# Loading a feed-forward layer's first weights a piece per attention pair, and the rest in one block behind the first batch's last v

## The chip, the cores and the metric

The program runs on one core of a Trainium2 chip. The metric is device time in microseconds; the time before is the median of 3 runs. Beside the runs there is one profiled execution, and every row below is from it. The engines are named as the profile names them: PE (matrix products and transposes; PEld is its weight load), DVE (vector), ACT (scalar), POOL, and SP, which issues all DMAs here; an engine's name with q behind it is its sequencer.

## The reference

Three layers follow one another on 4 x 576 tokens of width 512, all in float32:

```python
# attention: 4 batches x 8 heads, 576 tokens, head width 64
out_d     = softmax(q_d @ k_d.T / 8) @ v_d        # q, k, v averaged over 4 tokens each
out_local = softmax(mask(q @ k.T / 8)) @ v        # |i - j| < 4
x = repeat(out_d, 4) + out_local                  # -> [2304, 512]
# gated feed-forward, width 1536
x = (sigmoid(x @ w_gate) * (x @ w_val)) @ w_out
# soft mixture: 8 experts x 4 slots
logits = x @ phi;  d = softmax over tokens;  c = softmax over slots
slots = d.T @ x;  slots_out = relu(slots @ w1[e]) @ w2[e];  out = c @ slots_out
```

## The kernel before

**Staging.** The kernel's program is one list of steps, `head` and then `body`; every engine walks the same list and does its own part of each step, in that order. Attention works on pairs of heads (16 pairs, 4 to a batch). The head handles the four pairs of the first batch, in turns, and begins on pair 4; the body runs the gated layer over 18 tiles of 128 tokens, three chunks of 512 columns each (steps `gate (i, c)` and `val (i, c)`, 12 matrix products each), with the attention of the other batches, step by step, between them. Behind the body comes the mixture of experts.

**Steps of a pair p.** `Q0`, `Q1`, `K0`, `K1` transpose q and k; `S0`, `S1` are the local scores and `Sd` the pooled ones; `mx`, `ex`, `norm` (and `mxd`, `exd`, `norm_d`) the softmax; `PT` and `PdT` transpose probabilities; `pool_V` adds up v on POOL; `PVd`, `PV0` to `PV2` are the products with v. `PV` of pair p also waits until that pair's local v has landed in `vloc`.

**Weights of the gated layer.** w_gate and w_val are loaded in 12 pieces of 512 KB (`load_pieces` into `w_raw`, 128 partitions x 2 x 512 float32). Pieces 0 to 3 are chunk 0 (two for gate, two for val), 4 to 7 chunk 1, 8 to 11 chunk 2. Each is split into a high part (`w_hi`, a copy on ACT) and a low part (`w_lo`, a subtraction on DVE). `gate (0, c)` waits for the first 4c + 2 low parts, `val (0, c)` for 4c + 4.

**w_out.** It is loaded in 12 pieces of 256 KB into four stages (`load_wo_piece`, L498); `WT f` transposes piece f on PE (L909) and copies it on ACT, `GP f` multiplies it with phi, `GS` gathers four of them. Piece f + 4 may be loaded when `WT f` is done.

**SP's queue.** SP walks the step list as well (`sync_step`): after `Q1` and `K1` of a pair it loads q and k of the next, after `pool_V` the v to be pooled (`v4`), after `PV2` the local v of the next pair (six DMAs, L468 to L474). A load stands in SP's order behind all that is issued, or waited for, ahead of it. The extra loads of the head are in the function at the end of the kernel:

```python
if s == ("S1", 0):
    load_pieces(sp, range(0, 3))
if s[0] == "PV2" and s[1] < 3:
    load_pieces(sp, range(3 * s[1] + 3, 3 * s[1] + 6))
```

So pieces 0 to 2 come ahead of q and k of pair 2, pieces 3 to 5 behind the local v of pair 1, 6 to 8 behind that of pair 2, 9 to 11 behind that of pair 3. Pieces 0 to 5 of w_out are loaded within the first pair's steps.

The step lists of the turns (TURN, FIRST_TURNS, HEAD_TURN, LAST_TURN) give the order in the head; `program_steps` writes the body. In the head a turn splits one piece (`w_hi` and `w_lo`); the last turn has two more `w_hi`. The body opens with xs 0 (tile 0 split into high and low parts), WT 2, WT 3, w_lo 4, w_lo 5, w_hi 6, w_hi 7, mx0 and mx1 of pair 4, gate (0, 0).

Of the kernel before, what the change touches and what calls it, by code (L numbers as in the profile page):

```python
# [30 lines left out]
               PV0 PV1 PV2""")  # L31
HEAD_TURN = """S0+ S1+ w_hi norm norm_d PT0 PT1 PT2 mx0+ mx1+ PdT0 PdT1 Sd+ PVd pool_V+ Q++ ex+ K++ mxd+ exd+ w_lo
               PV0 PV1 PV2"""
LAST_TURN = """S0+ S1+ w_hi norm norm_d PT0 PT1 PT2 PdT0 PdT1 w_lo PVd w_hi w_hi PV0 PV1 PV2"""

UNITS = ("Q0", "Q1", "K0", "K1", "S0", "S1", "Sd", "PdT0", "PdT1", "PVd", "PT0", "PT1", "PT2", "PV0", "PV1", "PV2",
         "WT", "GP", "GS", "TR", "LG", "LS", "ELT", "SL")
# [19 lines left out]
def program_steps(tiles, chunks, groups, batch_tokens, pairs, heads_of, w_pieces, wo_pieces):  # L57

    turns = [*zip((-2, -1, 0), FIRST_TURNS)] + [(p, HEAD_TURN) for p in range(1, heads_of - 1)] + \
            [(heads_of - 1, LAST_TURN)]
    head = attention_steps(turns, 0, heads_of + 1)
    done = set(head)
    att = [s for s in attention_steps([(p, TURN) for p in range(heads_of - 2, pairs)], heads_of, pairs) if s not in done]
    f0 = sum(s[0] == "GP" for s in head)
    split = {name: sum(s[0] == name for s in head) for name in ("w_hi", "w_lo")}
    start = [("xs", 0), ("WT", f0), ("WT", f0 + 1)]
    for n in range(split["w_lo"], 8):
        if n >= split["w_hi"]:  # L70
            start.append(("w_hi", n))
        if n < 6:
            start.append(("w_lo", n))
    start += [("mx0", heads_of), ("mx1", heads_of)]
    att = [s for s in att if s not in start]


    t0 = tiles - 3
    ff = [(name, (i, c)) for i in range(t0) for c in range(chunks) for name in ("gate", "val")]
    ff += [(name, (i, 0)) for i in range(t0, tiles) for name in ("gate", "val")]  # L80
    for c in range(1, chunks):
        ff += [("gate", (t0, c)), ("val", (t0, c)), ("gate", (t0 + 1, c)), ("gate", (t0 + 2, c)), ("val", (t0 + 1, c)),
               ("val", (t0 + 2, c))]
    place_of = {s: n for n, s in enumerate(ff)}


    after = {n: [] for n in range(len(ff) + 12)}

    def put(n, *steps):
        after[n] += steps  # L90


    marks = [(0, 3)]
    for b in range(1, pairs // heads_of):
        first_tile = b * batch_tokens // P
        k = att.index(("PV2", heads_of * (b + 1) - 1)) + 1
        marks.append((k, place_of[("gate", (first_tile, 0))] - 3))
    marks.append((len(att), marks[-1][1]))
    for (k0, n0), (k1, n1) in zip(marks, marks[1:]):
        for k in range(k0, k1):  # L100
            put(n0 + (k - k0) * (n1 - n0) // max(k1 - k0, 1), att[k])

    for n in range(6, w_pieces):
        if n >= 8:
            put(n // 2 - 4, ("w_hi", n))
        put(n // 2 - 3, ("w_lo", n))

    for f in range(f0, wo_pieces):
        n = f - f0 + 1
        if f >= f0 + 2:  # L110
            put(n - 1, ("WT", f))
        put(n, ("GP", f))
        if f % 4 == 3:
            put(n + 1, ("GS", f // 4))
    for i in range(1, tiles):

        put(place_of[("gate", (i, 0))] - 2 if i < t0 else place_of[("gate", (t0 - 1, 0))] + i - t0, ("xs", i))
    for i in range(t0):
        for c in range(chunks):
            put(place_of[("val", (i, c))] + 1, ("TR", (i, c)))  # L120
    for g, (first, size) in enumerate(groups):
        n = place_of[("val", (first + size - 1, chunks - 1))]
        if first + size < t0:
            for at, name in ((2, "LG"), (3, "LS"), (5, "ELT"), (6, "SL")):
                put(n + at, (name, g))

    last_c, g = chunks - 1, len(groups) - 3
    n = place_of[("gate", (t0, 0))]
    for at, *those in ((1, ("LG", g)), (2, ("LS", g)), (3, ("ELT", g), ("TR", (t0, 0)), ("SL", g)), (5, ("TR", (t0 + 2, 0)))):
        put(n + at, *those)  # L130
    for c in range(1, last_c):
        n = place_of[("gate", (t0, c))]
        put(n + 2, ("TR", (t0, c)))
        put(n + 5, ("TR", (t0 + 2, c)))
    n = place_of[("gate", (t0, last_c))]
    for at, *those in ((2, ("TR", (t0, last_c))), (3, ("LG", g + 1)), (4, ("LS", g + 1), *[("TR", (t0 + 1, c)) for c in range(chunks)]),
                       (5, ("ELT", g + 1), ("LG0", g + 2), ("TR", (t0 + 2, last_c)), ("SL", g + 1)),
                       (6, ("LG", g + 2)), (7, ("LS", g + 2)), (8, ("ELT", g + 2)), (9, ("SL", g + 2))):
        put(n + at, *those)
    body = []  # L140
    for n, s in enumerate(ff):
        body.append(s)
        body += after[n]
    for n in range(len(ff), len(ff) + 12):
        body += after[n]
    return head, start + body
# [36 lines left out]
def build(nc, q, k, v, w_gate, w_val, w_out, phi, w1, w2, out):  # L183
# [26 lines left out]
    FK = FF // P  # L210
# [16 lines left out]
    head, body = program_steps(TILES, FC, GROUPS, S, PAIRS, HP, len(w_pieces), FK)  # L227
# [12 lines left out]
    with ctx:  # L240
# [3 lines left out]
        def sem(name):  # L244
            return ctx.enter_context(nc.semaphore(name))
# [71 lines left out]
        WO_STAGES = KT  # L317
# [52 lines left out]
        w_hi = sem("w_hi")  # L370
        w_lo = sem("w_lo")
# [57 lines left out]
        def wait_unit(eng, s):  # L429
            eng.wait_ge(unit_ready, at[s][0] + 1)  # L430
# [57 lines left out]
        def load_pieces(sp, of):  # L488
            for i in of:
                c, m, kk = w_pieces[i]  # L490
                src = (w_gate, w_val)[m][kk * P:(kk + WK) * P, c * CW:(c + 1) * CW].rearrange("(k p) n -> p k n", p=P)
                sp.dma_start(w_views(i)[0], src).then_inc(w_in[i], 16)


        def load_wo_piece(sp, f):
            if f >= WO_STAGES:
                wait_unit(sp, ("WT", f - WO_STAGES))
            sp.dma_start(wo_stage[f % WO_STAGES], w_out[f * P:(f + 1) * P, :]).then_inc(wo_in[f % WO_STAGES], 16)  # L498
# [47 lines left out]
        def sync_step(sp, s):  # L546
            name, arg = s
            if name == "Q1" and arg + 1 < PAIRS:
                wait_unit(sp, s)
                load_pair_qk(sp, arg + 1, "q")  # L550
            elif name == "K1" and arg + 1 < PAIRS:
                wait_unit(sp, s)
                load_pair_qk(sp, arg + 1, "k")
            elif name == "PV2" and arg + 1 < PAIRS:
                wait_unit(sp, s)
                load_v_local(sp, arg + 1)
            elif name == "WT" and arg + WO_STAGES < FK:
                load_wo_piece(sp, arg + WO_STAGES)
            elif name == "pool_V" and arg + 1 < PAIRS:
                sp.wait_ge(vd_done, arg + 1)  # L560
                load_v_pooled(sp, arg + 1)
# [567 lines left out]
        @block.sync  # L1129
        def _(sp):  # L1130
            load_pair_qk(sp, 0, "q")
            load_pair_qk(sp, 0, "k")
            for f in range(2):
                load_wo_piece(sp, f)
            sp.dma_start(phi_sb[:, :, :], phi.rearrange("(k p) s -> p k s", p=P)).then_inc(phi_in, 16)
            for s in head:
                sync_step(sp, s)
                if s == ("K1", 0):
                    load_v_pooled(sp, 0)
                    for f in range(2, WO_STAGES):  # L1140
                        load_wo_piece(sp, f)
                    load_v_local(sp, 0)

                if s == ("S1", 0):
                    load_pieces(sp, range(0, 3))
                if s[0] == "PV2" and s[1] < 3:
                    load_pieces(sp, range(3 * s[1] + 3, 3 * s[1] + 6))
            for s in body:
                sync_step(sp, s)

            wait_free(sp, *[(f"PV{u}", PAIRS - 1) for u in range(3)])
            load_wo_tail(sp)
            for i in range(FIRST):
                wait_place(sp, place_of_tile(i))
                load_tile(sp, i)
            for i in range(FIRST, N_TILES):
                n = place_of_tile(i)
                if n < WO_SLOTS:
                    sp.wait_ge(sin_ready, 1)
                else:  # L1160
                    gone = n - WO_SLOTS
                    sp.wait_ge((w1_used, w2_used)[gone // 2 % 2], gone // 4 + 1)
                load_tile(sp, i)
            for i in range(TILES):
                sp.wait_ge((out_evac_a, out_evac_v)[i % 2], i // 2 + 1)
                sp.dma_start(out[i * P:(i + 1) * P, :], outs[:, i, :]).then_inc(out_saved, 16)
            sp.wait_ge(out_saved, 16 * TILES)
# [76 lines left out]
```

## Time and profile before

| what | us |
|---|---|
| median of 3 runs | 601.73 (600.63 to 601.77) |
| the profiled execution, its own time | 600.79 |
| its span | 599.0 |
| PE busy in the span | 550.9 (92%) |
| DVE busy | 224.4 (37%) |
| ACT busy | 200.1 (33%) |
| POOL busy | 100.7 (17%) |
| chain that ended last: PE | 83% of the span |
| chain that ended last: DMA | 6% |

The span is what the profile's own clock covers; 1.8 us of the execution's time lie around it. A line of the timeline has the start, the duration, the engine, the line of the kernel, the operation, the tile written and read, the count of instructions merged, and in brackets the idle time of the engine before it and what ended that.

### The profile page before, as it was taken

Reading aid. Unit: us, or ns where it says so; the run is one execution under the profiler, and the core shown is the slowest. Engines: PE = TensorE matmul, PEld = TensorE weight load, DVE = VectorE, ACT = ScalarE, POOL = GpSimd, SP = SyncE. Lnnn points to the kernel's source line nnn. Section 1 sums busy time; section 2 is a strip of 40 time slices with the busy share of each in tenths; the row PEclk is TensorE's granted clock in tenths of the full one; section 3 lists DMA queues with packets and bytes.
Section 4 is the critical chain, followed back from the end, with each engine's and each line's share of the span. In section 5 each row is a group of like instructions: output and inputs, shape, how many; then the busy total and the mean of one; then the engine's idle time right before and its main releaser. Section 6 shows DMA issues by size and latency. Waiting matters only on the chain.

```text
span 599.0 us, 11279 instructions
## 1 busy us (share of the span) xinstructions
PE 550.9 (92%) x4486; PEld 413.8 (69%) x4486; DVE 224.4 (37%) x500; ACT 200.1 (33%) x514; POOL 100.7 (17%) x171
## 2 busy tenths in 40 slices
PE   5686899999999999999999999999999999968963
PEld 4575776776878778777777877787787777833422
DVE  3487752525535252434326243542212221130003
ACT  4355653343433424242333334133223211130103
POOL 7655012232221212112120302110000000000000
PEclk9779799999999999999999999999999999999988
DMA  9879522211311111202120110101703256589958
GB/s 201 209 198 230 177 80 69 65 40 42 82 40 42 41 42 36 46 20 53 27 48 20 50 33 21 23 3 34 267 1 109 103 207 257 202 313 394 399 197 315
DMA packets 86707, 70.97 MB, mean 118 GB/s; under 512 B 61312, under 2 KB 65920, under 8 KB 86656
## 3 DMA queue, kind: packets, MB, share of 16 engines
q1 hardware_dynamic: 86656, 70.25, 38.0%
q8 instruction: 36, 0.59, 0.4%
q14 instruction: 15, 0.12, 0.1%
HBM read 65.52 MB, written 4.72 MB: 117 GB/s over the span
## 4 chain that ended last, share of the span: by engine, by line
PE 83%; DMA 6%; DVE 5%; issue 2%; ACT 2%; SPq 1%; DVEq 0%
PE gateb L946 26%; PE valb L946 25%; PE unitb L954 4%; PE unitb L903 3%; DMA ew_low<-in_moe_w_dram 3%; PE unitb L859 3%; PE unitb L866 2%; PE unitb L968 2%; PE unitb L985 2%; PE unitb L894 2%; PE unitb L874 2%; DMA qtok<-in_q_dram 2%; PE unitb L1029 2%; PE unitb L881 1%; PE unitb L909 1%
## 5 line engine op out<-in xcount | busy, mean ns | idle before, releaser
L946 PE MATMUL gateb<-w_hl,xhl 128*128 128x512 f32 x648 | 162.8, 400 | 0.0
L946 PE MATMUL valb<-w_hl,xhl 128*128 128x512 f32 x648 | 162.1, 399 | 0.0
L946 PEld LDWEIGHTS gateb<-w_hl,xhl 128*128 128x128 f32 x648 | 118.7, 189 | 33.0 <-issue 9.1
L946 PEld LDWEIGHTS valb<-w_hl,xhl 128*128 128x128 f32 x648 | 118.6, 188 | 23.9 <-issue 0.2
L665 ACT ACTIVATE hid<-gateb 128x512 f32<-128x512 f32 x54 | 32.3, 598 | 170.9 <-PE gateb L946 170.9
L785 DVE SCALAR_TENSOR_TENSOR hid<-hid,valb 128x512 f32<-128x512 f32 x54 | 37.1, 688 | 128.7 <-PE valb L946 128.6
L583 POOL TENSOR_TENSOR vd<-v 72x256 f32<-72x256 f32 x16 | 12.7, 793 | 172.9 <-PE unitb L887 168.0
L594 ACT ACTIVATE hT<-unitb 128x512 f32<-128x512 f32 x54 | 32.0, 597 | 21.2 <-PE unitb L954 21.2
L768 DVE TENSOR_TENSOR xraw<-unitb,outd 128x192 f32<-128x192 f32 x43 | 15.0, 356 | 55.8 <-PE unitb L903 55.6
L954 PE MATMUL unitb<-ident,hid 128*128 128x128 f32 x216 | 33.3, 278 | 2.5 <-DVE hid L785 1.7
L954 PEld LDWEIGHTS unitb<-ident,hid 128*128 128x128 f32 x216 | 24.3, 140 | 7.7 <-issue 4.1
L903 PE MATMUL unitb<-probT,vloc 70*64 70x64 f32 x516 | 22.2, 231 | 4.6 <-DMA vloc<-in_v_dram 4.6
L903 PEld LDWEIGHTS unitb<-probT,vloc 70*64 70x64 f32 x516 | 18.2, 141 | 11.7 <-issue 10.9
L894 PE MATMUL unitb<-ident,prob 128*70 128x128 f32 x123 | 20.5, 282 | 3.9 <-DVE prob L747 3.9
L777 DVE TENSOR_TENSOR xhl<-xraw,xhl 128x512 fp32r<-128x512 f32 x18 | 12.8, 710 | 28.6 <-ACT xhl L594 28.6
L866 PEld LDWEIGHTS unitb<-kT,qT 64*64 64x64 f32 x488 | 17.8, 143 | 5.3 <-issue 5.0
L866 PE MATMUL unitb<-kT,qT 64*64 64x70 f32 x488 | 20.5, 235 | 0.3 <-ACT kT L594 0.3
L752 DVE COPY probT<-unitb 70x384 f32<-70x384 f32 x13 | 7.2, 553 | 34.5 <-PE unitb L894 34.5
L578 POOL TENSOR_TENSOR kd<-kd,kT 128x144 f32<-128x144 f32 x32 | 19.2, 599 | 2.5
L594 ACT ACTIVATE qT<-unitb 128x384 f32<-128x384 f32 (+1 forms) x30 | 11.1, 414 | 24.7 <-PE unitb L859 24.7
L578 POOL TENSOR_TENSOR qd<-qd,qT 128x144 f32<-128x144 f32 x32 | 18.9, 590 | 2.5
L575 POOL TENSOR_TENSOR qd<-qT 128x144 f32<-128x144 f32 x16 | 9.3, 580 | 59.3 <-ACT qT L594 59.2
(174 smaller groups left out, 666.7 us busy)
## 6 DMA issues: line engine op xcount, KB each, us to landing
ew_low<-in_moe_w_dram SPq DMA_DIRECT2D x19, 1024.0 KB, 13.7
ew_high<-in_moe_w_dram SPq DMA_DIRECT2D x13, 1024.0 KB, 7.9
qtok<-in_q_dram SPq DMA_DIRECT2D x32, 144.0 KB, 2.8
ktok<-in_k_dram SPq DMA_DIRECT2D x32, 144.0 KB, 3.0
v<-in_v_dram SPq DMA_DIRECT2D x32, 144.0 KB
out_dram<-outs SPq DMA_DIRECT2D x18, 256.0 KB, 3.0
vloc<-in_v_dram SPq DMA_DIRECT2D x32, 112.0 KB
xraw<-in_moe_w_out_dram SPq DMA_DIRECT2D x12, 256.0 KB, 3.6
```

The costliest lines, as they stand in the source:

```text
L578: nc.gpsimd.tensor_tensor(dst, dst, src[j], ALU.add).then_inc(step if j == 2 else done, 1)
L594: return nc.scalar.activation(dst, src, ACT.Copy, scale=scale)
L665: nc.scalar.activation(hid[:, i % NH, c * CW:(c + 1) * CW], gateb[n % 2][:, :], ACT.Tanh, scale=0.5)\
L768: nc.vector.tensor_tensor(dst.rearrange("p (g j) -> p g j", j=POOL), ub[:, 0:3 * QT].rearrange("p (g j) -> p g j", j=POOL), up, ALU.add).t ...
L777: nc.vector.tensor_tensor(xhl[:, arg % NX, 1, :, :], xraw[:, :, tok:tok + P], xhl[:, arg % NX, 0, :, :].bitcast(F32), ALU.subtract).then_i ...
L785: nc.vector.scalar_tensor_tensor(out=here, in0=here, scalar=1.0, in1=valb[n % 2][:, :], op0=ALU.add, op1=ALU.mult).then_inc(hid_done, 1)
L859: last = nc.tensor.transpose(ub[:, (t - t0) * TT:(t - t0 + 1) * TT], tok[:, t, :, :].rearrange("p h d -> p (h d)"), ident[0:TT, 0:TT])
L866: last = mm(ub[rows, (t - t0) * KW:(t - t0 + 1) * KW], qT[rows, t * QT:(t + 1) * QT], kT[rows, key_start(t):key_start(t) + KW], start=True ...
L894: last = nc.tensor.transpose(ub[0:KW, j * P:(j + 1) * P], prob[:, arg % 2, 3 * u + j, :], ident[:])
L903: last = mm(ub[rows, j * QT:(j + 1) * QT], vloc[:, t, h, :], probT[:, t, h * QT:(h + 1) * QT], start=True, stop=True)
L946: last = mm(bank[:, :], xhl[:, i % NX, x, kk, :], w_hl[:, c, m, w, kk, :], start=j == 0, stop=j == len(order) - 1)
L954: last = nc.tensor.transpose(ub[:, j * P:(j + 1) * P], hid[:, i % NH, f * P:(f + 1) * P], ident[:])
```

## The change

The head loads fewer weights ahead of its attention, and the rest in one block:

- Behind S1 of pair 0 come pieces 0 and 1; behind PV2 of pairs 0 and 1 one piece each (2 and 3). Each is loaded a turn before the turn that splits it.
- Behind PV2 of pair 2, and so behind the local v of pair 3, come pieces 4 to 11 and pieces 2 to 5 of w_out, in the order 4, 5, wo 2, 6, 7, wo 3, 8, 9, wo 4, 10, 11, wo 5. Pieces 2 to 5 of w_out are no longer loaded within the first pair's steps.
- The last turn of the head has one w_hi, no longer three. The body opens with xs 0, w_hi 4, w_lo 4, w_hi 5, w_lo 5, mx0, mx1. Pieces 6 and 7 are split behind gate (0, 0), 8 and 9 behind val (0, 0), 10 and 11 behind gate (0, 1).
- WT 2 and WT 3 go behind gate (0, 0) and behind val (0, 0).

```diff
-LAST_TURN = """... PdT0 PdT1 w_lo PVd w_hi w_hi PV0 PV1 PV2"""
+LAST_TURN = """... PdT0 PdT1 w_lo PVd PV0 PV1 PV2"""
...
-    start = [("xs", 0), ("WT", f0), ("WT", f0 + 1)]
-    for n in range(split["w_lo"], 8):
-        if n >= split["w_hi"]:
-            start.append(("w_hi", n))
-        if n < 6:
-            start.append(("w_lo", n))
+    split = sum(s[0] == "w_lo" for s in head)
+    start = [("xs", 0)]
+    for n in range(split, 6):
+        start += [("w_hi", n), ("w_lo", n)]
...
     for n in range(6, w_pieces):
-        if n >= 8:
-            put(n // 2 - 4, ("w_hi", n))
-        put(n // 2 - 3, ("w_lo", n))
+        put(n // 2 - 3, ("w_hi", n), ("w_lo", n))
...
-        if f >= f0 + 2:
-            put(n - 1, ("WT", f))
+        put(n - 1, ("WT", f))
...
-            elif name == "WT" and arg + WO_STAGES < FK:
+            elif name == "WT" and 2 <= arg < FK - WO_STAGES:
                 load_wo_piece(sp, arg + WO_STAGES)
...
                 if s == ("K1", 0):
                     load_v_pooled(sp, 0)
-                    for f in range(2, WO_STAGES):
+                    load_v_local(sp, 0)
+
+                if s == ("S1", 0):
+                    load_pieces(sp, range(0, 2))
+                if s[0] == "PV2" and s[1] < 2:
+                    load_pieces(sp, range(s[1] + 2, s[1] + 3))
+                if s == ("PV2", 2):
+                    load_pieces(sp, range(4, 6))
+                    for f in range(2, 6):
                         load_wo_piece(sp, f)
-                    load_v_local(sp, 0)
-
-                if s == ("S1", 0):
-                    load_pieces(sp, range(0, 3))
-                if s[0] == "PV2" and s[1] < 3:
-                    load_pieces(sp, range(3 * s[1] + 3, 3 * s[1] + 6))
+                        if f < 5:
+                            load_pieces(sp, range(2 * f + 2, 2 * f + 4))
```

## Rows read from the trace of the kernel before

**Rows 1.** The page, part 2: busy tenths and granted clock in 40 slices.

```profile
PE   5686899999999999999999999999999999968963
...
PEclk9779799999999999999999999999999999999988
```

**Rows 2.** The chain that ended last, in order of time: start, us, what.

```profile
16.64 9.93 DMA qtok<-in_q_dram
...
48.39 2.80 DMA vloc<-in_v_dram
...
60.45 1.65 DMA vloc<-in_v_dram
...
553.61 16.73 DMA ew_low<-in_moe_w_dram
```

**Rows 3.** Timeline from 18 to 27 us: SP's k load, PE around its gap.

```profile
18.48 6.14 SPq L463 DMA_DIRECT2D ktok<-in_k_dram  x2
...
21.96 0.95 PE L874 MATMUL valb<-kd,qd 64*64 64x144 f32 x12 [0.41 <-POOL kd L578]
...
26.70 1.15 PE L859 MATMUL unitb<-ident,qtok 96*128 96x96 f32 x6 [3.79 <-DMA qtok<-in_q_dram]
```

**Rows 4.** Windows of 2 us: busy us of each engine (instructions), PE's clock, DMA share, GB/s.

```profile
18.00:20.00 2.00, 2.00 (x20) 1.51 (x16) 1.35 (x3) 0.39 (x1) 1.84 (x4) 0.51 1.07 394
...
22.00:24.00 2.00, 0.92 (x12) 0.65 (x12) 1.65 (x3) 0.82 (x1) 0.00 (x0) 1.00 1.18 149
...
28.00:30.00 2.00, 2.00 (x28) 1.78 (x28) 0.26 (x1) 2.00 (x9) 1.42 (x3) 0.50 0.37 120
...
52.00:54.00 2.00, 1.84 (x57) 1.63 (x52) 1.95 (x5) 1.18 (x3) 1.84 (x5) 1.00 1.05 406
...
62.00:64.00 2.00, 1.77 (x34) 1.80 (x35) 0.54 (x2) 0.38 (x1) 0.00 (x0) 0.50 0.77 264
```

**Rows 5.** Timeline from 44 to 62 us: SP's loads ahead of local v, and PE.

```profile
44.17 1.09 SPq L463 DMA_DIRECT2D ktok<-in_k_dram  x2
...
48.39 0.32 SPq L474 DMA_DIRECT2D vloc<-in_v_dram  x1
...
51.32 1.27 PE L903 MATMUL unitb<-probT,vloc 70*64 70x64 f32 x36 [1.21 <-DMA vloc<-in_v_dram]
...
54.05 3.02 SPq L463 DMA_DIRECT2D ktok<-in_k_dram  x2
...
58.12 0.71 PE L887 MATMUL unitb<-probdT,vd 72*64 72x144 f32 x8 [0.54 <-ACT probdT L594]
...
60.45 0.32 SPq L474 DMA_DIRECT2D vloc<-in_v_dram  x1
...
62.23 0.91 PE L903 MATMUL unitb<-probT,vloc 70*64 70x64 f32 x12 [3.40 <-DMA vloc<-in_v_dram]
```

**Rows 6.** Timeline from 64 to 84 us: PE at the body's start.

```profile
64.35 1.97 PE L909 MATMUL unitb<-ident,xraw 128*128 128x128 f32 x8
...
65.97 3.83 PE L946 MATMUL gateb<-w_hl,xhl 128*128 128x512 f32 x12
...
76.11 0.66 PE L909 MATMUL unitb<-ident,xraw 128*128 128x128 f32 x4
...
83.19 3.01 PE L946 MATMUL gateb<-w_hl,xhl 128*128 128x512 f32 x12
```

**Rows 7.** The tile w_raw: min/median/max ns, first and last start.

```profile
L594 ACT ACTIVATE w_hl<-w_raw x12: 1042/1051/1097, 21.8 to 73.2; 128x1024 fp32r<-128x1024 f32 x12
L773 DVE TENSOR_TENSOR w_hl<-w_raw,w_hl x12: 1206/1218/1765, 23.5 to 76.6; 128x1024 fp32r<-128x1024 f32 x12
```

**Rows 8.** Timeline: the same 36 score products in two turns.

```profile
30.90 2.37 PE L866 MATMUL unitb<-kT,qT 64*64 64x70 f32 x36
...
41.14 1.32 PE L866 MATMUL unitb<-kT,qT 64*64 64x70 f32 x36 [0.30 <-ACT kT L594]
```

**Rows 9.** A window of 15 us in the head, columns as in Rows 4.

```profile
30.00:45.00 15.00, 13.13 (x182) 11.18 (x179) 13.17 (x28) 8.03 (x23) 7.63 (x12) 0.73 0.73 198
```

More of the change, by code:

```diff
@@ L33 @@
                PV0 PV1 PV2"""
-LAST_TURN = """S0+ S1+ w_hi norm norm_d PT0 PT1 PT2 PdT0 PdT1 w_lo PVd w_hi w_hi PV0 PV1 PV2"""
+LAST_TURN = """S0+ S1+ w_hi norm norm_d PT0 PT1 PT2 PdT0 PdT1 w_lo PVd PV0 PV1 PV2"""
 UNITS = ("Q0", "Q1", "K0", "K1", "S0", "S1", "Sd", "PdT0", "PdT1", "PVd", "PT0", "PT1", "PT2", "PV0", "PV1", "PV2",
@@ L66, in program_steps @@
     f0 = sum(s[0] == "GP" for s in head)
-    split = {name: sum(s[0] == name for s in head) for name in ("w_hi", "w_lo")}
-    start = [("xs", 0), ("WT", f0), ("WT", f0 + 1)]
-    for n in range(split["w_lo"], 8):
-        if n >= split["w_hi"]:
-            start.append(("w_hi", n))
-        if n < 6:
-            start.append(("w_lo", n))
+    split = sum(s[0] == "w_lo" for s in head)
+    start = [("xs", 0)]
+    for n in range(split, 6):
+        start += [("w_hi", n), ("w_lo", n)]
     start += [("mx0", heads_of), ("mx1", heads_of)]
@@ L1139, in _ @@
                     load_v_pooled(sp, 0)
-                    for f in range(2, WO_STAGES):
-                        load_wo_piece(sp, f)
                     load_v_local(sp, 0)
                 if s == ("S1", 0):
-                    load_pieces(sp, range(0, 3))
-                if s[0] == "PV2" and s[1] < 3:
-                    load_pieces(sp, range(3 * s[1] + 3, 3 * s[1] + 6))
+                    load_pieces(sp, range(0, 2))
[4 more added lines that the diff above has]
+                    for f in range(2, 6):
+                        load_wo_piece(sp, f)
+                        if f < 5:
+                            load_pieces(sp, range(2 * f + 2, 2 * f + 4))
             for s in body:
```

## The prediction

> **What bounds the kernel now.** I began with the page's slices, to see where PE is not the bound. A slice is 15 us. From the sixth to the thirty-fifth PE is full at the full clock; it has holes in the first five (75 us), where the granted clock also drops, and in the last five [rows 1]. The change touches the first 85 us only. The later work follows PE: where PE reaches the body earlier, all behind it moves by as much, the loads of the experts' weights too, since SP issues them when PE's work has freed their places; the wait of 16.73 us for them at the end moves along and does not shrink [rows 2]. So the question is how much earlier PE gets through the head and the body's first chunk.
>
> Then I read the chain in order of time for what it says of DMA in the head. It names three transfers: q of pair 2, and the local v of pairs 2 and 3 [rows 2]. On PE's timeline they are three gaps: 3.79 us up to 26.70 [rows 3], 1.21 us up to 51.32 and 3.40 us up to 62.23 [rows 5]. The windows say what the DMA engines did ahead of each gap. At 18 to 20 us they moved 394 GB/s: weights, in rows of 2 KB. At 22 to 24 us they were as busy and moved 149, the 256-byte rows of q and k [rows 4]. So q of pair 2 stood behind weights that nobody needed yet, and SP's issue of k behind it took 6.14 us where 1.09 is enough for the same two DMAs in a later turn [rows 3, 5]. I read that as back-pressure of the full queue.
>
> **First gap.** Taken from in front of q of pair 2: pieces 2 to 5 of w_out (4 x 256 KB) and weight piece 2 (512 KB), 1.57 MB. At 394 GB/s [rows 4] that is 4.0 us. q landed at 16.64 + 9.93 = 26.6 [rows 2], so it would land at 22.6; PE is done with the work ahead at 21.96 + 0.95 = 22.9 [rows 3]. The gap goes nearly whole. Five issues leave SP's queue there too, which only helps. Bounds: 0 (if q is slow for another reason, as its 149 GB/s might say) and 3.79. I take 3.7: weights moved at 394 just ahead of it. What is late next is nothing on PE: the v to be pooled lands earlier as well, and the local v of pair 0 stands ahead of the pieces.
>
> **Second gap.** Pieces 3 to 5 had been moved well before the local v of pair 2 was issued, and 6 to 8 are issued behind it. It landed some 2.6 us after its last issue (48.39 + 0.32 to 51.32) [rows 5], and that issue stands behind pooled v, q and k on SP, which start only when POOL is done. The change takes none of that away. Bounds 0 and 1.21; I take 0.
>
> **Third gap.** Here pieces 6 to 8 (1.5 MB) go out just ahead of v, q and k: 406 GB/s at 52 to 54 us [rows 4], and the k issue takes 3.02 instead of 1.09 [rows 5]. With one piece there the 1.9 us go, so the last v issue ends at 58.8 instead of 60.77 and the data, 1.5 to 2.6 us behind it as in the two cases, is there at 60.3 to 61.4. PE is ready at 58.12 + 0.71 = 58.83. So 1.5 or more of the gap stays and about 1.9 goes. Bounds 0 and 3.40; I take 1.9.
>
> **WT 2 and WT 3.** Eight transposes leave the place ahead of the first gate product: the gate starts 65.97 - 64.35 = 1.62 us sooner. They come back between gate and val at the full clock, 0.66 for four as the profile models it [rows 6], or down to 0.45 as far as the next product lets them overlap: 0.9 to 1.3 us. Gain 0.3 to 0.7; I take 0.5.
>
> **The splitting.** DVE's part is eight w_lo of 1.22 us behind the head as before. ACT gets two more w_hi, 2.1 us, in the body [rows 7]. w_hi 4 and 5 lie under the first gate product (3.83 us [rows 6]), where ACT has only xs 0 to finish. Then ACT's order is: tanh of gate (0, 0), w_hi 6, w_hi 7, the copy of WT 2, w_hi 8 and 9, copies of GP 2 and WT 3, tanh of gate (0, 1). Queued behind the two w_hi is the copy that GP 2 on PE waits for: it ends about 0.7 + 2.1 + 0.6 = 3.4 us after gate (0, 0); PE comes to GP 2 after WT 2 and val (0, 0), 0.7 + 2.9 = 3.6 us. This is covered by 0.2 us only. Without cover it costs what is missing, up to 2.1. I take a loss of 0.4.
>
> **The block.** Eight pieces and four of w_out are 5.24 MB, 12.9 us at 406 GB/s [rows 4]. Its issue starts behind the local v of pair 3, at 58.8 less the 3.7 gained before, so at 55.1; some 2 us later it moves. Piece 5 is there at about 60, piece 7 (2.36 MB) at 63, piece 9 at 66, piece 11 at 70. PE starts gate (0, 0) at 65.97 - 3.7 - 1.9 - 1.6 = 58.8, so ACT, done with xs 0 at about that time, asks for piece 4 at 58.7, for 6 at 63.3, 7 at 64.4, 8 at 66, 11 at 72. Piece 4 lands near 58.5. All are just in time, and the small waits fall under gate (0, 0). The local v of pair 4 and all later loads now queue behind the block on SP; pair 4 needs its v only behind the whole of tile 0. Cost 0; bounds 0 and the slower rival below.
>
> The Trainium skill's page DMA: Bandwidth & Descriptors, section Where 436 GB/s comes from, says that transfers from HBM are bound at about 358 GB/s for a core; by that the block would take an estimated 14.6 us and piece 11 would come at 72, still in time, so the sum would not change by more than some tenths. The windows here differ, at 394 and 406 GB/s over 2 us, and the trace decides.
>
> **The clock.** Behind the first gap the granted clock is 0.50, the lower level of 1.2 GHz (28 to 30 us), and behind the third again (62 to 64 us) [rows 4]. The same 36 products took 2.37 us there and 1.32 at the full clock [rows 8], so one turn could win over 1 us on these alone. But in that turn DVE is busy 13.17 of 15 us [rows 9], so it would soon be the bound; and with a gap of 1.5 us left ahead of PV of pair 3 the clock may stay low there. Bounds: a loss of 1 (the drop falls on another stretch) to a gain of 3. I take 0.8, nearer to nothing because DVE is close.
>
> The Trainium skill's page TensorE: Matmul & The Clock Gate, Part 1, says that the throttled state is the default and only activity releases it. The rows agree as far as the low level stands behind each long gap. By that rule alone both stretches would come at full speed once the gaps are gone, which is the rival of a larger gain below.
>
> **Sum.** 3.7 + 0 + 1.9 + 0.5 - 0.4 + 0 + 0.8 = 6.5 us. From the profiled execution's own 600.79 that gives 594.3; it lay 0.94 below the median of the runs, so the forecast of the median is 595.2.
>
> **Rivals.**
> - *Only the first gap goes* (chance 0.14). SP's chain POOL, pooled v, q, k, local v sets when PV can start, and a PE that comes earlier just waits longer there; the body gives back a part. For it: the second gap stands without any piece in the way. Against it: the first gap moves the start of that chain too. 3.7 less 0.5 to 2.1: 598.5 to 600.1.
> - *Slower* (0.06). The block comes too late and ACT, in order, holds up PE. If it moved at the pace of the small rows, 149 to 200 GB/s [rows 4], piece 11 would land near 57 + 5.0 MB / 0.175 = 86; the copies and the softmax of pair 4 stand behind its split on ACT, and gate (0, 2), at 83.19 before [rows 6], would start near 90: 6 to 7 us slower, about 608. It decides below some 225 GB/s, where piece 11 lands near 79. Against it: pieces alone on the queue have moved at 394 to 406.
> - *The gain is spent again* (0.07). Both GP 2 and GP 3 wait for ACT and the low clock comes back in other turns: within 0.2% of 601.7, the resolution of a measurement of this kernel.
> - *Larger gain* (0.06). Full clock from 27 us on and at the first gate: 3 us instead of 0.8, the second gap gone too: 588 to 591.5.
>
> The forecast itself, 592 to 598, has 0.67. Faster by over 0.2% (below 600.5) is the forecast, the larger gain and the first rival: 0.87; no change 0.07, slower 0.06. The range from 589.8 to 600.1 takes in the first rival and half of the larger gain, and leaves out about 0.16.
>
> **What would show it.** After the change the gap ahead of the transposes of q of pair 2 is under 0.5 us, and no k issue in the head is over 2 us. The gap ahead of PV of pair 3 is 1 to 2 us, that of pair 2 about as before. gate (0, 0) starts near 59 and gate (0, 2) near 77, 6 to 7 us ahead of 83.19; from there to the end everything is shifted by the same amount. The 2 KB rows run in one stretch of 13 us at about 400 GB/s from 56 us on. Wrong it would be if ACT's w_hi in the body wait for their pieces, if PE waits at GP 2 or GP 3 for over 1 us, or if the low clock covers as much of the head as before.

## The result and the profile after

| | us |
|---|---|
| before, 4 runs | 601.31 (600.63 to 601.77) |
| changed kernel, 4 runs | 596.64 (594.65 to 597.21) |
| ratio, 95% interval | 0.9917 [0.9892, 0.9943] |
| profiled execution of before, of the changed kernel | 600.79, 594.65 |

The change makes the kernel 4.7 us faster by the medians, 6.1 us by the two profiled executions; that of the changed kernel was the fastest of its four runs. The forecast was 595.2 from a sum of 6.5 us.

The page of the changed kernel, part 2, PE and its clock by slices of 15 us:

```profile
PE   6787998999999999999999999999999999968963
...
PEclk9697999999999999999999999999999999999988
```

Against [rows 1] the slices 1, 2, 4 and 5 are a tenth fuller, the seventh is a tenth emptier, and from the eighth on PE's line is the same digit for digit. What the change does, it does in the first 77 us. The timeline there, with the lines that answer to [rows 3, 5, 6] (PE, and of SP the k loads, the pooled v of pair 4 and the last DMA for the local v of pair 3):

```profile
18.64 1.06 SPq L457 DMA_DIRECT2D ktok<-in_k_dram  x2
...
23.20 0.97 PE L868 MATMUL valb<-kd,qd 64*64 64x144 f32 x12 [1.75 <-POOL kd L572]
...
24.09 1.22 PE L853 MATMUL unitb<-ident,qtok 96*128 96x96 f32 x6
...
36.90 1.32 PE L860 MATMUL unitb<-kT,qT 64*64 64x70 f32 x36 [0.25 <-ACT kT L588]
...
46.77 1.27 PE L897 MATMUL unitb<-probT,vloc 70*64 70x64 f32 x36 [1.01 <-DMA vloc<-in_v_dram]
...
47.34 0.74 SPq L475 DMA_DIRECT2D v<-in_v_dram  x2
...
49.10 1.92 SPq L457 DMA_DIRECT2D ktok<-in_k_dram  x2
...
54.56 0.32 SPq L468 DMA_DIRECT2D vloc<-in_v_dram  x1
...
54.80 0.71 PE L881 MATMUL unitb<-probdT,vd 72*64 72x144 f32 x8 [0.54 <-issue]
...
56.35 0.57 PE L897 MATMUL unitb<-probT,vloc 70*64 70x64 f32 x12 [0.84 <-DMA vloc<-in_v_dram]
...
58.18 4.57 PE L940 MATMUL gateb<-w_hl,xhl 128*128 128x512 f32 x12 [0.55 <-ACT xhl L588]
...
66.22 0.66 PE L903 MATMUL unitb<-ident,xraw 128*128 128x128 f32 x4
...
77.00 3.01 PE L940 MATMUL gateb<-w_hl,xhl 128*128 128x512 f32 x12
```

PE no longer waits for q of pair 2, and the issue of k has gone from 6.14 us to 1.06. But PE now waits 1.75 us just ahead of that place, for POOL's pooled k (`kd`) of pair 1: a smaller gap has taken the place of the first. The gap at pair 2's v stands (1.01 us), that at pair 3's has shrunk from 3.40 to 0.84. The body then takes longer from gate (0, 0) to gate (0, 2). Put together by the starts of PE's work (scores of the next pair, then the two gates), with a second profile of the changed kernel from another execution (run c below):

| stretch up to | before | changed | changed, second profile |
|---|---|---|---|
| scores of pair 2 | 30.90 | 28.33 | 26.08 |
| scores of pair 3 | + 10.24 | + 8.57 | + 9.93 |
| scores of pair 4 | + 11.38 | + 11.07 | + 9.96 |
| gate (0, 0) | + 13.45 | + 10.21 | + 12.34 |
| gate (0, 2) | + 17.22 = 83.19 | + 18.82 = 77.00 | + 18.95 = 77.26 |

6.19 us are gained at gate (0, 2), and 6.1 at the end of the span. The two profiles of one kernel split them differently, by up to 2.3 us at a stretch, and agree at gate (0, 0) within 0.13 us; run c below takes that up.

The weights' block, in windows with the columns of [rows 4]:

```profile
62.00:64.00 2.00, 2.00 (x13) 1.64 (x12) 1.97 (x4) 1.22 (x2) 0.00 (x0) 1.00 1.02 390
64.00:66.00 2.00, 2.00 (x14) 1.40 (x15) 1.93 (x4) 1.76 (x3) 0.00 (x0) 1.00 1.05 400
66.00:68.00 2.00, 2.00 (x18) 1.59 (x15) 2.00 (x3) 1.43 (x2) 0.00 (x0) 1.00 1.05 386
```

It moves in one stretch near the rate that was assumed, beside a full PE: from 58 to 68 us 387 GB/s on average in this profile, 383 in the second.

### The profile page after: what moved, and what is told of

Same layout as the page of the kernel before. It is cut to its first block, busy times and chain, and to the rows that moved or that the text cites. A ratio compares the mean times of both kernels' runs of the same rounds, so it can differ in the third digit from the quotient of the medians.

```text
span 592.9 us, 11279 instructions
## 1 busy us (share of the span) xinstructions
PE 549.3 (93%) x4486; PEld 412.9 (70%) x4486; DVE 224.3 (38%) x500; ACT 200.1 (34%) x514; POOL 101.5 (17%) x171
## 4 chain that ended last, share of the span: by engine, by line
PE 83%; DMA 5%; DVE 4%; issue 2%; ACT 2%; POOL 1%; SPq 1%; POOLq 0%; ACTq 0%; DVEq 0%
PE gateb L940 26%; PE valb L940 25%; PE unitb L948 4%; PE unitb L897 3%; DMA ew_low<-in_moe_w_dram 3%; PE unitb L853 3%; PE unitb L860 2%; PE unitb L962 2%; PE unitb L979 2%; PE unitb L888 2%; PE unitb L868 2%; PE unitb L1023 2%; PE unitb L875 2%; PE unitb L881 1%; PE gateb L1041 1%
## 5 line engine op out<-in xcount | busy, mean ns | idle before, releaser
L588 ACT ACTIVATE probdT<-unitb 72x288 f32<-72x288 f32 x29 | 10.8, 405 | 24.0 <-PE unitb L875 24.0
```

Of the source, the lines that this page charges most:

```text
L588: return nc.scalar.activation(dst, src, ACT.Copy, scale=scale)
```

## The experiments

Each ratio is to runs of the kernel before on the same chip; the medians of before were 601.27 (e1 to e5), 601.30 (e6 to e8 and c) and 601.24 us (e9, e10).

**e1, the early part alone**, in the kernel before (the edits of e1 and e2 are shown in part). Behind PV2 of pair 1 stay pieces 6 to 8; behind that of pair 2 come pieces 2 and 3 of w_out, weight pieces 9 to 11, and pieces 4 and 5 of w_out.

```diff
-                    load_pieces(sp, range(0, 3))
+                    load_pieces(sp, range(0, 2))
...
-                if s[0] == "PV2" and s[1] < 3:
-                    load_pieces(sp, range(3 * s[1] + 3, 3 * s[1] + 6))
+                if s == ("PV2", 0):
+                    load_pieces(sp, range(2, 6))
```

> The kernel before, with only the early part of the change: pieces 2 to 5 of w_out leave the first pair's steps (they go among pieces 9 to 11), and weight piece 2 moves from behind S1 of pair 0 to behind PV2 of pair 0. The later loads (three or four pieces a pair) and the order of the splits stay. Theory: the gap ahead of q of pair 2 becomes a POOL wait of about 1.8 us, the products of pair 2 start 2.6 us sooner, the low clock ends sooner in that turn, and the gap of 3.4 us ahead of PV of pair 3 stays or grows: 2.5 to 4.5 us faster than before, 596.8 to 598.8. Rival (SP's chain ahead of local v takes back what the first gap gives): within 1 us of before. Rival (the whole gain is in the first gap and its clock): as fast as the change, about 596.6.

Measured: 599.27 us, 0.9966 [0.9950, 0.9981], between the theory and the first rival. The start of the scores of pair 3 was 5.2 us ahead (35.96 for 41.14), and most of it was lost to new waits (PE's timeline):

```profile
46.19 0.87 PE L859 MATMUL unitb<-ident,qtok 96*128 96x96 f32 x4 [3.36 <-DMA qtok<-in_q_dram]
...
61.08 0.91 PE L903 MATMUL unitb<-probT,vloc 70*64 70x64 f32 x12 [3.01 <-DMA vloc<-in_v_dram]
```

The first is q of pair 4, behind the four pieces that now stand ahead of it: the same fault in a later turn. Freed of its first wait the head runs into the next; this part alone is worth 2 us.

**e2, the late part alone**: the changed kernel with the early loads of before. Pieces 2 and 3 of w_out stand again behind the pooled v of pair 0, 4 and 5 behind WT 0 and WT 1; piece 3 behind PV2 of pair 1, pieces 4 to 11 behind that of pair 2.

```diff
-                    load_pieces(sp, range(0, 2))
+                    load_pieces(sp, range(0, 3))
```

> The changed kernel with the early loads of before: pieces 2 to 5 of w_out within the first pair's steps, weight pieces 0 to 2 behind S1 of pair 0, piece 3 alone behind PV2 of pair 1, pieces 4 to 11 in one block behind the local v of pair 3, and the new order of splits and WT. Theory: the first gap is back at 3.8 us with the low clock behind it, the one ahead of PV of pair 3 is about 1 us and no k issue there takes 3 us; the body's order costs about 1.5 us: 1.5 to 3 us faster than before, 598.3 to 599.8. Rival (the low clock ahead of the first gate product takes it all): no faster than before. Rival (all the gain is here): about 596.6.

Measured: 599.42 us, 0.9965 [0.9946, 0.9984], in the range of the theory for the time.

```profile
27.96 1.19 PE L853 MATMUL unitb<-ident,qtok 96*128 96x96 f32 x6 [4.61 <-DMA qtok<-in_q_dram]
...
60.71 0.57 PE L897 MATMUL unitb<-probT,vloc 70*64 70x64 f32 x12 [2.25 <-DMA vloc<-in_v_dram]
```

The first gap is back, with 4.61 us; the third is there with 2.25, where about 1 was expected. Each part is worth about 2 us, the two together 4.7 to 5.9.

**e4, local v of pair 0 behind pieces 0 and 1.**

```diff
                 if s == ("K1", 0):
                     load_v_pooled(sp, 0)
-                    load_v_local(sp, 0)
...
                     load_pieces(sp, range(0, 2))
+                    load_v_local(sp, 0)
```

> The changed kernel with the local v of pair 0 issued behind weight pieces 0 and 1 and no longer directly behind the pooled v of pair 0. Theory (the 256-byte rows of the local v are moved at the same time as the pooled v and delay it): POOL starts the first addition at about 12.3 us instead of 13.33, the wait of PE for kd falls from 1.75 to about 0.7 us, and the whole is up to 1 us faster than the change. Rival (pooled v is late because of q and k of pair 1 issued ahead of it): POOL starts at 13.3 as in the change, no difference.

Measured: 595.87 us, 0.9902 [0.9881, 0.9923], not to be told from the change. POOL's first addition in e4:

```profile
12.49 0.73 POOL L577 TENSOR_TENSOR vd<-v 72x256 f32<-72x256 f32 x1 [1.43 <-DMA v<-in_v_dram]
```

It starts at 12.49, against 13.33 in the change's first profile, about as the theory had it. But that doesn't show that the local v's rows delay the pooled v: in other profiles with the local v straight behind the pooled v, as in the change, the same addition starts anywhere from 12.38 (e7) to 13.33.

```profile
12.38 0.72 POOL L577 TENSOR_TENSOR vd<-v 72x256 f32<-72x256 f32 x1 [1.35 <-DMA v<-in_v_dram]
```

PE's wait for kd stayed at 1.75 us, against what was expected: PE's own work ahead of it came sooner too, at the full clock. The wait began and ended 0.6 us earlier.

**e5, rep's selects moved on POOL.**

```diff
-                if s == ("pool_V", 0):
+                if s == ("pool_V", 4):
```

> The changed kernel with POOL's seven selects that build rep (3.1 us, needed first by GS 0 in the body) moved from behind pool_V of pair 0 to behind pool_V of pair 4, where POOL is idle. Theory (the first gap now ends on POOL's chain, and the selects are in it): the wait of PE for kd of pair 1 goes, 1.75 us, and the turn starts that much sooner: 1.5 to 2.5 us faster than the change, about 594.6. Rival (q of pair 2 or the v chain on SP is late right behind it): the gap moves to DMA, under 0.5 us faster.

Measured: 593.92 us, 0.9870 [0.9847, 0.9894]: 2.7 us below the change by the medians (1.5 below its second set of runs, c). `rep` is a constant matrix that is first needed in the body; POOL builds it with seven selects (the affine_select of L1190). The first line is from the change, the others from e5:

```profile
16.09 3.08 POOL L1190 TENSOR_SCALAR_AFFINE_SELECT rep<-rep 128x128 f32<-128x128 f32 x7
```

```profile
21.33 0.95 PE L868 MATMUL valb<-kd,qd 64*64 64x144 f32 x12
...
24.87 1.32 PE L860 MATMUL unitb<-kT,qT 64*64 64x70 f32 x36 [0.25 <-ACT kT L588]
...
53.70 2.92 POOL L1190 TENSOR_SCALAR_AFFINE_SELECT rep<-rep 128x128 f32<-128x128 f32 x7
...
54.55 0.91 PE L897 MATMUL unitb<-probT,vloc 70*64 70x64 f32 x12 [3.27 <-DMA vloc<-in_v_dram]
```

The wait for kd is gone, so what had taken the first gap's place was POOL's queue, with 3.1 us of selects in it that nobody in the head needs. The scores of pair 2 start 3.5 us ahead of the change's 28.33, PV of pair 3 only 1.8 us ahead of its 56.35. Against the change's second profile (c, next) the two leads are 1.2 and 1.6 us. So part of the larger lead belongs to the low clock of the first profile, and what e5 itself gains at PV and by the medians is some 1.5 to 2.7 us.

**c, the changed kernel again.**

> The changed kernel itself, unaltered, for a second profile and more times beside the same runs of before. Theory: 4 to 6 us faster than before; the three gaps as in its first profile (1.7 to 1.8 us for kd of pair 1, 0.8 to 1.3 us for each local v), while the low clock lies on other stretches and moves single starts by up to 1 us.

Measured: 595.44 us, 0.9905 [0.9884, 0.9926]. The time is as expected, the profile was the surprise (SP and PE; the last line is from the kernel before):

```profile
22.54 0.95 PE L868 MATMUL valb<-kd,qd 64*64 64x144 f32 x12 [0.78 <-POOL kd L572]
23.42 0.71 PE L853 MATMUL unitb<-ident,qtok 96*128 96x96 f32 x6
...
26.08 1.32 PE L860 MATMUL unitb<-kT,qT 64*64 64x70 f32 x36 [0.25 <-ACT kT L588]
...
46.65 1.19 SPq L475 DMA_DIRECT2D v<-in_v_dram  x2
...
53.34 0.32 SPq L468 DMA_DIRECT2D vloc<-in_v_dram  x1
...
56.15 0.91 PE L897 MATMUL unitb<-probT,vloc 70*64 70x64 f32 x12 [3.54 <-DMA vloc<-in_v_dram]
```

```profile
52.27 0.76 SPq L481 DMA_DIRECT2D v<-in_v_dram  x2
```

The wait for kd is 0.78 us here, not 1.75, and the gap that was said to have shrunk is back: the same kernel has 0.84 us of waiting for the local v of pair 3 in one profile and 3.54 in the other. Yet PV of pair 3 starts at 56.35 and 56.15. In this execution the clock was full from 21 to 55 us and PE came early; in the other it was low from 24 to 31 us and from 48 to 55. The start of PV follows SP and not PE: it lies 9.5 us here, 9.0 there, 10.0 before (52.27 to 62.23) behind the issue of the pooled v of pair 4. That issue waits for POOL's additions for pair 3, and these for PE's PVd of pair 2, a turn earlier. Then q, k and six loads for the local v follow on SP, one after the other. The last of them ends at 53.66 here and at 54.88 there; the data is waited for until 2.5 us and 1.5 us after that.

**e6, SP's order changed**: local v ahead of the pooled v.

```diff
             for s in head:
-                sync_step(sp, s)
+                if s[0] != "pool_V" or s[1] == 0:
+                    sync_step(sp, s)
+                if s[0] == "PV2" and s[1] < 3:
+                    sync_step(sp, ("pool_V", s[1] + 1))
```

> The changed kernel with another order on SP in the head: the pooled v of pairs 2 to 4 is issued behind PV2's local v and no longer, with its wait for POOL, ahead of q, k and local v. Theory (what is left of the second and third gap is SP's own chain, POOL's additions, then pooled v, q, k, local v): the local v of pairs 2 and 3 lands ahead of its product, the waits of 1.01 and 0.84 us for it and that of 0.50 us for k go: 1.5 to 2.5 us faster than the change, about 594.6. Rival (these waits are the transfers' own time behind the weights): they stay, no difference. Rival (the pooled v is late now): POOL waits for v and PE for vd, slower than the change.

Measured: 592.37 us, 0.9858 [0.9830, 0.9886], the best with e7, and more than expected. All waits for the local v are gone, so they were SP's order, not the transfers' time. The scores of pair 2 start at 25.87, as in c (26.08), and the clock is full in both from there to 55 us, but PV of pair 3 starts 5.3 us ahead of c's 56.15. POOL now waits for the pooled v, up to 3.20 us, as the second rival had it, but PE nowhere waits for vd. PE up to the body:

```profile
50.86 0.55 PE L897 MATMUL unitb<-probT,vloc 70*64 70x64 f32 x12
...
52.70 3.00 PE L940 MATMUL gateb<-w_hl,xhl 128*128 128x512 f32 x12 [0.59 <-ACT xhl L588]
...
57.41 0.63 PE L903 MATMUL unitb<-ident,xraw 128*128 128x128 f32 x4 [1.71 <-DMA xraw<-in_moe_w_out_dram]
...
72.72 3.01 PE L940 MATMUL gateb<-w_hl,xhl 128*128 128x512 f32 x12
```

gate (0, 0) starts 5.5 us ahead of the change, and PE now meets the block: it waits for piece 2 of w_out, and the stretch to gate (0, 2) takes 20.0 us instead of 18.8 or 19.0.

**e7, both e5 and e6.**

> The changed kernel with both: SP's order as in the run before it in this list, and rep's seven selects on POOL behind pool_V of pair 4. With the selects moved alone the first gap went (the products of pair 2 started at 24.87 us, not 28.33), but 3.27 us came back as a wait for the local v of pair 3. Theory: the new order on SP takes that wait away, so the two gains add up and some of the lost one comes back: 588.5 to 591.5. Rival (DVE or ACT bound the turns by now): no better than the selects alone, about 593.9.

Measured: 592.30 us, 0.9854 [0.9832, 0.9875]. The theory failed: the gains don't add up. The rival's figure, the 593.9 of the selects alone, wasn't met either. Against e6 the scores of pair 2 start 1.6 us earlier (24.31), gate (0, 0) 0.4 (52.30) and gate (0, 2) 1.2 later (73.89, 21.6 us after gate (0, 0)). So most of the lead is gone within the turns, and the body takes the rest. In the body ACT waits for pieces of the block (2.22 us for piece 4, 1.41 and 1.11 for two later ones) and PE for ACT's copies. That the body is the bound now is read off these waits; no run shows it by itself.

**e8, the block a turn later.**

```diff
-                if s == ("PV2", 2):
+                if s == ("PV2", 3):
```

> The changed kernel with the whole block one turn later, behind the local v of pair 4 and not of pair 3, some 6 us later on SP. It asks for the price of a block that comes too late, the slower rival of the prediction. Theory (ACT is in order and holds up the copies that PE waits for): ACT waits for piece 4 some 6 us, piece 11 lands near 77.5, gate (0, 2) starts at 81 to 82 and not at 77: 4 to 5.5 us slower than the change, 600.5 to 602, about as before. Rival (the body has cover enough, since gate (0, 2) needs only pieces 0 to 9): under 1.5 us slower than the change.

Measured: 602.45 us, 1.0028 [1.0004, 1.0052], 5.8 to 7.0 us slower than the change, somewhat more than the theory's 4 to 5.5. ACT and PE:

```profile
64.15 1.06 ACT L588 ACTIVATE w_hl<-w_raw 128x1024 fp32r<-128x1024 f32 x1 [6.54 <-DMA w_raw<-in_moe_w_gate_dram]
```

```profile
66.69 1.08 PE L903 MATMUL unitb<-ident,xraw 128*128 128x128 f32 x4 [5.95 <-DMA xraw<-in_moe_w_out_dram]
...
82.78 2.98 PE L940 MATMUL gateb<-w_hl,xhl 128*128 128x512 f32 x12
```

The block's lateness comes through nearly whole: gate (0, 2) is 5.8 us later than in the change. Another 1.6 us of this profile are a low clock in the body, which the last section takes up.

**e9, e6 with the first 1.3 MB of the block a turn earlier; e10, the same with e5's edit too.**

```diff
+                if s == ("PV2", 1):
+                    load_pieces(sp, range(4, 6))
+                    load_wo_piece(sp, 2)
                 if s == ("PV2", 2):
-                    load_pieces(sp, range(4, 6))
                     for f in range(2, 6):
-                        load_wo_piece(sp, f)
+                        if f > 2:
+                            load_wo_piece(sp, f)
```

> The kernel with SP's new order in the head, and besides the first 1.3 MB of the block (pieces 4 and 5 and piece 2 of w_out) a turn earlier, behind piece 3 and the local v of pair 2. In the run with the new order alone the first gate product began at 52.70 us, but PE then waited 1.71 us for piece 2 of w_out and 0.80 us for a copy behind a late w_hi, and gate (0, 2) began 20.0 us later, not 18.8. Theory (the block is what is late now): these waits go, gate (0, 2) comes 1.5 to 2.5 us sooner against gate (0, 0), and the time is 1 to 2.5 us below that run, 590 to 591.4. Rival (the 1.3 MB delay q, k and local v of the last turn, as the weights did before the change): a wait for them on PE of over 1 us, no faster.

> As the run before it in this list, with rep's selects on POOL behind pool_V of pair 4 too. Theory: POOL's selects no longer matter once SP's order has changed (592.30 against 592.37 without this), so no difference from the run before it beyond 0.5 us. Rival (they were hidden by the late block): 1 to 2 us faster than it.

Measured: 593.82 us, 0.9881 [0.9862, 0.9900], and 592.95 us, 0.9871 [0.9853, 0.9888]. The rival held for e9:

```profile
42.95 3.47 SPq L457 DMA_DIRECT2D ktok<-in_k_dram  x2
...
53.67 0.67 PE L897 MATMUL unitb<-probT,vloc 70*64 70x64 f32 x12 [3.69 <-DMA vloc<-in_v_dram]
```

The 1.3 MB stand ahead of q, k and local v. PE waits 3.69 us for the local v of pair 3, and PV starts 2.8 us behind e6's 50.86. From gate (0, 0) to gate (0, 2) it takes 19.7 us, 0.3 less than in e6, where 1.5 to 2.5 was expected. e10 has the same wait, of 3.61 us. Its difference to e9 is smaller than their spread and decides nothing; nor do the times show e9 slower than e6, only not faster.

## Why the prediction was right, and where not

**The direction, the size and the end** hold: 6.5 us were forecast, 6.1 measured between the profiles, 4.7 and 5.9 between medians. gate (0, 2) was put near 77 and starts at 77.00 and 77.26. Everything behind moves along to 0.1 us in the first profile and to 0.4 in the second. But the terms did not come out as the sum has them. The starts of the work on PE and SP give them so (us, the two profiles of the change against before):

| part of the sum | forecast | first | second |
|---|---|---|---|
| first gap, up to the transposes of q of pair 2 | 3.7 | 2.6 | 3.3 |
| from there to the issue of the pooled v of pair 4 (second gap, clock) | 0.8 | 2.3 | 2.3 |
| from that issue to PV of pair 3 (third gap) | 1.9 | 1.0 | 0.5 |
| from PV of pair 3 to gate (0, 2) (WT, splitting, block) | 0.1 | 0.3 | -0.2 |
| sum | 6.5 | 6.2 | 5.9 |

That the sum came so near is in part luck: two terms were too large, and a stretch in which little was expected made up for them.

**First gap, 3.7 us: mis-sized, by a step that was wrong.** That the weights ahead of q of pair 2 were the cause is shown by e2, where they are back and the gap is 4.61 us. But "what is late next is nothing on PE" is false. The sum took PE's work ahead of the gap as fixed at 22.9; one piece of it moved, Sd of pair 1, from 21.96 to 23.20 and 22.54, since POOL's kd was late. One cause is shown: POOL has rep's selects in its queue, and with them moved the wait is gone (e5). Nor did the pooled v land earlier: POOL's first addition starts at 13.33 and 12.94, and at 12.30 before. Why is open; e4 does not settle it.

**Second gap, 0: right.** 1.01 and 0.71 us are left of 1.21, for the reason given, SP's order, which e6 removes.

**Third gap, 1.9 us: the right place, the wrong quantity.** The price of the gap was reckoned on PE's timeline, as if its width were the loss. The width is only what PE is ahead of the chain on POOL and SP: 0.84 or 3.54 us in one kernel. The chain itself, from the issue of the pooled v to PV, became 0.5 to 1.0 us shorter (10.0 to 9.5 and 9.0), not 1.9; its beginning moved by 4.9 and 5.6 us with the earlier turns. The issue of k did shrink, from 3.02 us to 1.92 and 1.15. But with the 1.5 to 2.6 us that the prediction itself put between the last issue and the data, 0.8 to 1.9 us of the gap would go, and the sum took the upper end. Of the signs named for it, a gap of 1 to 2 us is in neither profile, and no k issue over 2 us holds in the first only (2.40 us in the second).

**WT and the splitting, together 0.1 us: right**, as far as two profiles tell. From PV of pair 3 to gate (0, 0) it is 1.8 and 2.2 us, 3.7 before, and the body gives 1.6 and 1.7 back. PE does not wait at GP 2 or GP 3.

**The block, 0: right**, at 383 to 387 GB/s over ten us. ACT's w_hi did wait for pieces in the first profile (0.97 us for piece 4), which was named as a sign of being wrong; the wait lies under the first gate product and costs PE nothing. The rate stands above the 358 GB/s that the Trainium skill's page DMA: Bandwidth & Descriptors (Where 436 GB/s comes from) gives as the bound from HBM, which it reckons as one core's half of a rate that two cores share. The margin was as thin as the working said: e6 starts 5.5 us sooner and waits at once, and e8, 6.5 us late at ACT, loses 5.8. So the slower rival's mechanism is real and its condition did not hold here.

**The clock, 0.8 us: not shown as a term of its own.** Between the transposes of q of pair 2 and the issue of the pooled v of pair 4 the change gains 2.3 us in both profiles, more than the 0.8. Before, the clock was low for 13.7 us of the two turns there, up to PVd of pair 2; in the changed kernel for 6.7 us and for none. Yet the two profiles take the same 23.2 us for the stretch, and the 2.3 us that the second is ahead at the scores of pair 2 is gone at gate (0, 0): where PV waits for a chain on POOL and SP, a faster PE gains only by what it starts that chain earlier, 0.7 us here. How much of the 2.3 us is the clock stays open. The same is why the rival "larger gain" had no ground, and why "only the first gap goes" was half right: in e1 the early gain is taken back by later waits.

## What to carry to other kernels

A wait on the bounding engine has a place and a width, and only the place says what is limiting: work out the chain that releases it from where that chain starts, and price the change by how much the chain gets shorter. When a transfer is taken from the front of a queue, list who stands right behind it on that queue and on the engine that it feeds; here that was POOL, with work in its queue that could stand later. Take a second profile of one kernel before a difference of starts is put down to an edit: here the starts in the head of one kernel differed by up to 2.3 us. And a block that is moved back has a due time: a turn later cost about 6 us, and a quarter of it a turn earlier made the next local v late and gained nothing.

## What was not expected of the hardware

Two executions of one kernel had the low clock, 0.50 of 2.4 GHz, on different stretches of the head, though PE's program is the same: from 21 us on about 24 to 31, 48 to 55 and 58 to 62 us in one, 55 to 62 us in the other. A wait of PE alone doesn't decide it either. In the first profile the wait of 1.75 us for kd has the low clock behind it, and the 36 scores of pair 2 take 2.37 us. In e4 and e8, behind waits of 1.75 and 1.76 us, they take 1.32.

In some profiles a low stretch also lies in the body. In e9 it is at 119 us, where the change has none (windows, columns as in [rows 4], first e9, then the change):

```profile
119.00:123.00 4.00, 4.00 (x12) 3.22 (x12) 0.69 (x1) 0.84 (x2) 1.58 (x2) 0.59 0.23 75
```

```profile
119.00:123.00 4.00, 4.00 (x34) 2.98 (x31) 1.24 (x2) 2.10 (x6) 2.68 (x3) 1.00 0.01 4
```

From the start of gate (0, 2) to that of the last gate product it takes 434.1 us in e9 and 432.4 in both profiles of the change. It is 432.4 in each of the profiles without a low stretch in the body (before, e1, e2, e5, e6) and 434.0 in the others that have one (e4, e7, e8, e10), so one such stretch cost 1.6 us, whatever the edit. What decides where these stretches fall is open.
